# A gated delta rule with two feed-forward layers: small products of 64 output rows split into two of 32, and one transpose to the lanes in place of three

## The reference

```python
k_n = k / (np.linalg.norm(k, axis=-1, keepdims=True) + 1e-06)
for t in range(S):
    y[:, :, t] = np.einsum('bhd,bhde->bhe', q[:, :, t], state)
    v_old = np.einsum('bhde,bhd->bhe', state, kt)
    state = state + bt[:, :, :, None] * np.einsum('bhd,bhe->bhde', kt, vt - v_old)
...
h = np.maximum(x @ w_in, 0.0);  x = h * h @ w_out
gate = 1.0 / (1.0 + np.exp(-(x @ w_gate)));  out = (gate * (x @ w_val)) @ w_last
```

## Time and profile before

| | |
|---|---|
| median of 3 runs | 1164.22 us (1162.77 to 1165.63) |
| the profiled execution, its own time | 1156.84 us |
| its span, first to last instruction | 1155.1 us |
| TensorE busy / weight loads busy | 91% / 48% |
| VectorE / ScalarE busy | 51% / 38% |
| mean granted TensorE clock | 0.948 |

### The profile page before, as it was taken

How to read it: one execution, slowest core, us unless ns; L and a number is a source line. 1 busy time by engine, 2 the same in 40 slices (tenths; PEclk the granted TensorE clock), 3 DMA queues, 4 the chain that set the end, 5 groups by cost and what they waited for, 6 DMA issues and landing times.

```text
span 1155.1 us, 23126 instructions
## 1 busy us (share of the span) xinstructions
PE 1048.1 (91%) x9957; PEld 551.9 (48%) x9957; DVE 587.5 (51%) x1100; ACT 439.3 (38%) x752; POOL 14.0 (1%) x27
## 2 busy tenths in 40 slices
PE   3498579988988998899889999999999999999997
PEld 1274246545644664466446544444444444444443
DVE  7848943793489159716952445524233342422422
ACT  4551244425434443445344488222222222132221
POOL 0000000000000000000000000000000000000000
PEclk7699689988999998899889999999999999999999
DMA  9423002400230043004200051101001010010000
GB/s 299 74 71 42 1 2 43 70 28 2 70 43 29 2 87 53 2 16 70 110 2 2 1 181 39 55 1 55 0 0 54 0 54 0 0 54 0 27 0 27
DMA packets 54851, 48.12 MB, mean 42 GB/s; under 512 B 45424, under 2 KB 49392, under 8 KB 54384
## 3 DMA queue, kind: packets, MB, share of 16 engines
q1 hardware_dynamic: 54336, 46.67, 15.8%
q10 hardware_dynamic: 432, 0.23, 0.1%
HBM read 37.45 MB, written 9.44 MB: 41 GB/s over the span
## 4 chain that ended last, share of the span: by engine, by line
PE 75%; DVE 21%; issue 2%; ACT 2%; DVEq 0%; POOL 0%; POOLq 0%
PE psum L526 59%; DVE attn L876 4%; DVE attn L874 4%; PE psum L401 3%; DVE attn L894 2%; PE psum L463 2%; PE psum L476 2%; PE psum L451 2%; PE psum L436 2%; PE psum L413 2%; DVE work L916 2%; PE psum L497 2%; DVE work L935 1%; DVE attn L881 1%; PE psum L425 1%
## 5 line engine op out<-in xcount | busy, mean ns | idle before, releaser
L526 PE MATMUL psum<-work,w 128*128 128x512 f16 x1728 | 410.8, 394 | 34.7 <-DVE work L916 30.7
L526 PE MATMUL psum<-work,attn 128*128 128x512 f16 x1944 | 419.9, 379 | 0.1
L526 PEld LDWEIGHTS psum<-work,attn 128*128 128x128 f16 x1944 | 190.1, 98 | 229.8 <-DVE work L935 0.6
L526 PEld LDWEIGHTS psum<-work,w 128*128 128x128 f16 x1728 | 167.0, 101 | 245.8 <-DVE work L916 39.1
L607 ACT ACTIVATE work<-work 128x512 f16<-128x512 f32 (+1 forms) x264 | 156.2, 624 | 147.3 <-DVE work L1097 139.8
L1097 DVE SCALAR_TENSOR_TENSOR work<-psum,work 128x512 f32<-128x512 f32 x72 | 49.8, 691 | 269.7 <-PE psum L526 258.8
L607 ACT ACTIVATE attn<-psum 32x512 f32<-32x512 f32 (+4 forms) x168 | 81.5, 500 | 108.7 <-PE psum L401 59.6
L607 ACT ACTIVATE work<-psum 128x512 f32<-128x512 f32 x96 | 57.0, 594 | 151.6 <-PE psum L526 151.2
L916 DVE SCALAR_TENSOR_TENSOR work<-work 128x512 f16<-128x512 f16 x96 | 66.2, 689 | 85.1 <-ACT work L607 83.7
L607 ACT ACTIVATE work<-psum,scal 128x512 f32<-128x512 f32 x72 | 49.4, 687 | 138.6 <-PE psum L526 137.8
L910 DVE TENSOR_TENSOR attn<-attn,psum 64x384 f32<-64x384 f32 x48 | 26.5, 552 | 88.1 <-PE psum L476 69.6
(11 more groups left out here) (77 smaller groups left out, 573.6 us busy)
## 6 DMA issues: line engine op xcount, KB each, us to landing
attn<-in_kt SPq DMA_DIRECT2D x24, 192.0 KB, 4.3
attn<-in_v SPq DMA_DIRECT2D x6, 768.0 KB, 4.7
attn<-in_kn SPq DMA_DIRECT2D x6, 768.0 KB, 7.0
x_spill<-work SPq DMA_DIRECT2D x6, 768.0 KB, 3.5
xt<-x_spill SPq DMA_DIRECT2D x6, 768.0 KB, 4.9
y_out<-work SPq DMA_DIRECT2D x6, 768.0 KB, 3.6
attn<-in_qt SPq DMA_DIRECT2D x20, 192.0 KB, 4.6
work<-in_w_out SPq DMA_DIRECT2D x1, 3072.0 KB, 21.7
```

Source lines behind the costliest of these rows:

```text
L526: m = mm(dst, x, z, start=first and i == 0, stop=last and i == len(a) - 1)
```

## The change

In every fill except `mid`, `off` and `xt`, the product of 64 output rows becomes two of 32: the stationary operand's 64 columns are cut in two halves h = 0, 1, and the moving operand is streamed once for each. The output rows are 0 to 31, 64 to 95, 32 to 63, 96 to 127 in turn, so a pair's four products stand on four different column strips of the array: two tiles become four, and a fill's instructions double (x64). For the lower half (h = 1) of a `kk` fill the two column blocks of the moving operand are taken in the other order, so that the diagonal block stands in columns 0 to 31 of `gp` in all four strips, and the block that `mid` needs stands in columns 32 to 63. So `to_lanes` is one transpose of 128 partitions. In stages 1 to 4 it is at step 21. The line numbers of the changed kernel are some higher: L401 is L407 there, L436 L441, L451 L457, L463 L469, L476 L482, L526 L532, L835 L839.

```diff
-L_NORM, L_DIAG, L_COEF, L_START, L_COL = 0, 3, 4, 12, 14
+L_NORM, L_DIAG, L_COEF, L_START, L_COL = 0, 1, 2, 10, 12
...
-LANES_AT, NORM_AT, START_AT = (19, 20, 21), 22, 24
+LANES_AT, NORM_AT, START_AT = 21, 22, 24
...
+            def part_of(i, h):
+                return slice(CH * i + BL * h, CH * i + BL * (h + 1))
...
-                for j, i in itertools.product(range(HALF), range(2)):
+                for j, h, i in itertools.product(range(HALF), range(2), range(2)):
                     u = PAIRS * c + HALF * x + j
                     rows = features_of(i)
                     k = kt_s[rows, g % 2, u, :]
-                    last = mm(to[steps_of(i), CH * j:CH * (j + 1)], k, pq[rows, u, i, :] if kind == "qk" else k,
-                              start=True, stop=True)
+                    if kind == "qk":
+                        moving = pq[rows, u, i, :]
+                    elif h == 0:
+                        moving = k
+                    else:
+                        moving = k.rearrange("p (h t) -> p h t", t=BL)[:, ::-1, :]
+                    last = mm(to[part_of(i, h), CH * j:CH * (j + 1)], k[:, part_of(0, h)], moving, start=True, stop=True)
...
-                    last = mm(to[CH * i:CH * i + BL, BL * j:BL * (j + 1)], gp[rows, u, 0:BL], e_s[rows, u, BL:CH],
+                    last = mm(to[CH * i:CH * i + BL, BL * j:BL * (j + 1)], gp[rows, u, BL:CH], e_s[rows, u, BL:CH],
...
-                for j, i in itertools.product(range(HALF), range(2)):
+                for j, h, i in itertools.product(range(HALF), range(2), range(2)):
                     p, u = HALF * x + j, PAIRS * c + HALF * x + j
-                    last = mm(to[steps_of(i), HD * j:HD * (j + 1)], pq[:, u, i, :], us[:, p, i, :],
+                    last = mm(to[part_of(i, h), HD * j:HD * (j + 1)], pq[:, u, i, part_of(0, h)], us[:, p, i, :],
                               start=True, stop=True)
...
-            def to_lanes(g, n):
-
-                if n == 0:
-                    for c, x in itertools.product(range(NC), range(2)):
-                        wait_taken(dve, "kk", g, c, x)
-                rows, b = ((slice(0, P), 0), (slice(BL, 2 * BL), BL), (slice(3 * BL, P), BL))[n]
-                lane(V.transpose(lane_g[rows].rearrange("p (s t) -> p t s", t=BL),
-                                 gp[rows, :, b:b + BL].rearrange("p u t -> p t u")), g, L_NORM + n)
+            def to_lanes(g):
+
+                for c, x in itertools.product(range(NC), range(2)):
+                    wait_taken(dve, "kk", g, c, x)
+                lane(V.transpose(lane_g.rearrange("p (s t) -> p t s", t=BL),
+                                 gp[:, :, 0:BL].rearrange("p u t -> p t u")), g, L_NORM)
```

More of the change, by code:

```diff
@@ L380, in steps_of @@
                 return slice(CH * i, CH * (i + 1))
+            def part_of(i, h):
+                return slice(CH * i + BL * h, CH * i + BL * (h + 1))
             def features_of(i):
                 return slice(CH * (1 - i), CH * (1 - i) + HD)
-            def features_padded(i):
-                return slice(CH * (1 - i), CH * (2 - i))
             def grams(kind, g, c, x):
@@ L433, in k_state @@
                 to = bank("ks", g, c, x)
-                for j, i in itertools.product(range(HALF), range(2)):
+                for j, h, i in itertools.product(range(HALF), range(2), range(2)):
                     p = HALF * x + j
-                    last = mm(to[steps_of(i), HD * j:HD * (j + 1)], kt_s[features_of(i), g % 2, PAIRS * c + p, :],
+                    last = mm(to[part_of(i, h), HD * j:HD * (j + 1)],
+                              kt_s[features_of(i), g % 2, PAIRS * c + p, part_of(0, h)],
                               us[features_of(i), p, i, :], start=True, stop=True)
@@ L448, in solve @@
                 to = bank("dr", g, c, x)
-                for j, i in itertools.product(range(HALF), range(2)):
+                for j, h, i in itertools.product(range(HALF), range(2), range(2)):
                     u = PAIRS * c + HALF * x + j
-                    last = mm(to[steps_of(i), HD * j:HD * (j + 1)], e_s[steps_of(i), u, :], v_s[steps_of(i), u, :],
+                    last = mm(to[part_of(i, h), HD * j:HD * (j + 1)], e_s[steps_of(i), u, part_of(0, h)], v_s[steps_of(i), u, :],
                               start=True, stop=True)
@@ L473, in state @@
                 to = bank("su", g, c, x)
-                for j, i in itertools.product(range(HALF), range(2)):
+                for j, h, i in itertools.product(range(HALF), range(2), range(2)):
                     p = HALF * x + j
-                    last = mm(to[features_padded(i), HD * j:HD * (j + 1)], kn_s[steps_of(i), PAIRS * c + p, :],
+                    last = mm(to[part_of(1 - i, h), HD * j:HD * (j + 1)], kn_s[steps_of(i), PAIRS * c + p, part_of(0, h)],
                               us[steps_of(i), p, i, :], start=True, stop=True)
@@ L1012, in stage @@
                     if s == 0 and step == OPEN:
-                        for n in range(3):
-                            to_lanes(0, n)
+                        to_lanes(0)
                         norms(0)
@@ L1051, in stage @@
                     if s == 0 and step == XSPLIT_AT + 1:
-                        for n in range(3):
-                            to_lanes(1, n)
+                        to_lanes(1)
                         norms(1)
                     if 0 < s < GROUPS - 1:
-                        if step - d in LANES_AT:
-                            to_lanes(s + 1, LANES_AT.index(step - d))
+                        if step == LANES_AT + d:
+                            to_lanes(s + 1)
                         if step == NORM_AT + d:
```

## The result

The changed kernel takes 1173.47 us (median of 6 runs, 1168.94 to 1177.25) where the kernel before takes 1165.68 in the runs beside it: 1.007 times as long, 95% interval 1.0048 to 1.0091. It is slower by 7.8 us; 1135.7 was forecast, 28.5 us faster. Its profiled execution took 1174.46 us, with a span of 1172.6 at a mean clock of 0.942.

What follows compares the result with a forecast made beforehand. TensorE was taken to bound a middle stage's first half, DVE the second. Transposes 4.2 + 4.3, fills 16.8 + 2.5 and grams 0.7 sum to 28.5 us: 1164.2 - 28.5 = 1135.7 us, own range 1127 to 1144 (0.62), whole range to 1160.

Steps and rivals of the forecast that it cites:

- Transposes, end of stage 0 (4.3): Two of three `to_lanes` transposes dropped before the `mid` of stage 1, where DVE is busy without waits: 4.3 us saved.
- Transposes, start (4.2): Two of three transposes of 2.10 us dropped at the head of stage 0's eliminations, for which TensorE waits: 4.2 us saved.
- Fills (16.8 + 2.5): `ks`, `dr`, `yy`, `su`: round 59.4 to 46 ns, 0.21 us a fill; 16.8 us in stages 1 to 5, 2.5 in stage 0.
- Grams (0.7): Gram fills stay at 60 ns a round by the stream; only the first load shortens, 0.03 us in 24 fills: 0.7 us.
- rival 2: Instructions fed too slowly, at best 15.9 ns a product: +0.07 us for 118 fills, 1164 us, no change; chance 0.08.
- The clock (left out, 3 us either way): TensorE's clock halves once or twice a stage after waits for DVE, which stay; not in the sum, 3 us either way.
- Rival 3: Strips of one row group hinder each other in the fills: 1186 us, or 1228 if streams alternate; chance 0.13 including a costly swap.
- a costly swap: Swapped blocks in `kk` double the swapped tiles' stream, at most 21 us; costed at nothing; chance 0.13 together with rival 3.

Runs made afterwards that it cites:

- e3: The changed kernel with all fills split but `kk` not swapped, so the three transposes stay: 1176.91 us, 1.0122 times the kernel before.
- e13: The changed kernel with every split kept, the second pair of `yy` and `su` fills one step later from stage 1 on: 1160.53 us, 0.9973 times before.
- e4: The kernel before plus 48 split fills, then 12 of 64-row products, over zeros ahead of the second feed-forward layer; no total given, a block takes 3.67 us.
- e8: The changed kernel, with SP waiting for the last of the first four `kk` fills before issuing other input transfers: 1174.2 us in a single execution.

## Why the prediction was wrong, point by point

- **Transposes, end of stage 0 (4.3): right.** 4.4 us by e3 against the changed kernel. That the two in each of stages 1 to 4 cost nothing is right too: the DVE half takes 46.4 to 46.8 us, and 46.5 to 46.7 before.
- **Transposes, start (4.2): right as work, lost as time.** The wait for L880 fell from 32.8 to 28.6 us as forecast, and a hole of 3.59 us ahead of it, in four fills that the sum held to run as before or better, took it back (e3, which keeps the three transposes and has the hole as well, has its first `mid` at 55.3). Rows before the change could not show it: those fills took 4.05 us there for 128 products, one block. The doubled fills need a second block just when the queue of the input transfers takes 99.8% of the 16 DMA engines' time (changed kernel, 6 to 17 us).
- **Fills (16.8 + 2.5): undersized where the supply keeps up, 0.25 us a fill and not 0.21.** Products start 10.9 ns apart, 11.6 was forecast, and a fill is 0.82 us, not 0.85. A round of some 43.5 ns is just above the 40 that the stream of 48 columns costs, so the 6 ns on top were too much.
- **Grams (0.7): near.** (1.10 - 0.216)/63 = 14.0 ns, a round of 56; a fill starts 1.03 us before the next one, against 1.08.
- **The step that failed: the sum has no term for the supply of instructions, because rival 2 was put away.** What stood in its place is 33.5 us of holes in the profiled execution, more than the forecast gain of 28.5. I took the densest distance in the trace, 15.9 ns in `off`, as evidence on the rate at which products can be fed, and put the rival away because tiles explained it. But `off` is 128 products, exactly one block, with feed-forward products on either side: it shows how fast a stock is used, not how fast it is refilled. The rate of refilling is 28.7 ns, and a fill of 64 products, for 0.25 us less of time, uses 64 x 28.7 = 1.84 us of supply instead of 0.92. Rival 2 was priced per product (+0.07 us a fill); what counts is the run. Four split fills take 3.3 us and 1.5 to 2.5 us of holes, 4.8 to 5.8 in all, where before they took 4.27. Two take 1.64 without a hole.
- **The four middle stages, summed.** The table of their TensorE halves (`mid` to second `xt`), changed kernel and before:

```profile
166.60:231.40 64.80, 60.24 (x1698) 36.99 (x1699) 19.95 (x38) 30.68 (x65) 0.87 (x1) 0.94 0.22 46
277.80:341.70 63.90, 60.66 (x1697) 37.12 (x1698) 19.85 (x37) 30.62 (x65) 0.81 (x1) 0.93 0.23 47
388.10:454.50 66.40, 61.92 (x1698) 37.12 (x1699) 21.53 (x43) 30.59 (x65) 0.91 (x1) 0.92 0.25 50
500.90:564.80 63.90, 60.28 (x1698) 36.80 (x1699) 19.91 (x38) 30.53 (x65) 0.84 (x1) 0.95 0.19 35
```

```profile
482.00:544.70 62.70, 62.70 (x1058) 40.81 (x1058) 24.29 (x40) 30.68 (x65) 0.85 (x1) 0.95 0.19 35
```

  In sum 259.0 us now and 251.3 before, +7.7. By the busy time of each line in these stretches, the feed-forward products take 151.0 us now and 145.2 before, and `mid` 13.4 and 14.5: +4.7 together, by half clock. (Half clock holds for twice (1 - PEclk) of a stretch, 33.7 us now and 25.1 before, and costs half of the 8.6 more, +4.3.) The holes are +15.8, of which 15.6 in `yy` and `su` (4.6, 3.2, 4.4 and 3.4). The grams take 0.6 less. The 64 fills of `ks`, `dr`, `yy` and `su` take 57.2 us and took 69.5, 12.3 less: that makes +7.6. It is 0.19 us a fill and not 0.25, since a fill that is cut by a hole starts anew (the last 5 products of L482 above take 0.28 us), and since some waits are too short for the list, as in the L482 above that took 1.15 us and not 0.88. On average the supply would do: a half holds about 1698 products in 64 us, one per 38 ns. Only their bunching exceeds it, as e13 showed.
- **The clock (left out, 3 us either way): undersized.** It is +4.7 us in the four TensorE halves alone. The forecast had the clock fall only after waits for DVE; the changed kernel's profile has a half-clock stretch right behind a hole in stage 3 (the hole of 1.80 us ends at 446.75), where before, in the same place from 425.0 to 445.0 us, stands at 1.00:

```profile
440.00:447.00 7.00, 4.63 (x262) 3.49 (x260) 1.10 (x2) 2.18 (x7) 0.00 (x0) 1.00 0.08 28
447.00:450.40 3.40, 3.40 (x12) 1.16 (x10) 3.09 (x10) 0.00 (x0) 0.00 (x0) 0.50 0.83 135
```

- **Rival 3: refuted.** It needed 18 ns and more between starts; `yy`, whose four strips use all 128 rows, has 10.9, as short as `su`, whose strips share rows by twos. By the rule of the Trainium skill in "TensorE: Matmul & The Clock Gate", "The mechanism", a weight load would not overlap with the products of its own rows; the trace disagrees, with the same 10.9 ns.
- **The chances.** 0.13 for slower rested on rival 3 and a costly swap; rival 2, with 0.08, held the true cause, but at a price that only made up for the transposes. Priced by the length of a run it would have stood on the side of slower.

## What to carry to other kernels

Doubling the instructions of a TensorE product costs instruction supply, and that shows only once a run of short instructions outlasts the stock: look in the trace for the longest dense run, not the densest one, and compare the change with it (here products 29.7 ns apart ran for hundreds without a hole, and the supply gave one per 28.7). Up to one block of short products between long ones came free; there the split brought 0.25 us per fill. Applied only there it took 1153.5 us, against 1164.5 before and 1173.5 for the split everywhere; with the 20 dummy products these three are 1142.4, 1164.1 and 1166.3. A saving on DVE at the start of the program was worth nothing here, since TensorE ahead of it had to wait for its instructions.

## What the runs showed of the hardware that was not expected

- TensorE's instructions came in blocks of 256, one in 3.47 to 4.02 us and 3.67 on average (e4), when nothing else moved. A block under way among the input transfers made a hole of 3.59 us instead of 1.27 (e8).
- After 29 us of little demand, 288 short instructions ran before the first hole (e4), so the stock ahead was between one and two blocks.
- Four tiles of 32 output rows, with 48 streamed columns, start 10.9 ns apart, also when all four read the same 128 rows. The Trainium skill ("TensorE: Matmul & The Clock Gate", "Wait — 56ns, not 53.3ns?") says that start-to-start never falls below about 25 ns; the trace disagrees.
